# One product over 384 columns for a head's turn in place of three over 128, in a fused attention and mixture-of-experts kernel

## The chip, the cores and the metric

The kernel runs on one core of a Trainium2 chip. The metric is the device time of one launch in microseconds, from several runs; lower is better. One more execution was recorded by the profiler, and all rows below come from it.

## The reference

Attention with a threshold, then experts whose outputs are all summed with weights:

```
scores = scale * (q @ k.T)                      # 4 batches, 8 heads, 576 x 64
thresh = max(scores, -1) - tau
scores = where(scores >= thresh, scores, -1e9)
attn = exp(scores - max(scores))
attn = attn / (sum(attn) + 1e-9)
x = (attn @ v) -> 2304 tokens x 512             # heads side by side
p = probs / (sum(probs) + 1e-9)                 # 2304 x 4
out = sum over e of p[:, e] * (relu(x @ w1[e]) @ w2[e])   # 512 -> 1024 -> 512
```

All inputs and the output are float32.

## The kernel before

**Tokens in chunks.** The 2304 tokens are cut into chunks of 384, 640, 640 and 640. For each chunk the attention is computed for all 8 heads, and then four experts run over it. Attention of the first chunk runs alone; that of a later chunk runs among the experts' products of the chunk before it.

**Units.** Heads are taken in pairs; each head of a pair is a turn. The query rows of a pair are cut into units of 128, numbered through the whole kernel (131 of them). The first chunk has 4 pairs, 8 turns and 24 units, three for each turn (the code calls these pairs solid; `SOLID` is 24). The first 27 units (`LONE`) are done before the first expert product is allowed to start.

**Steps of a unit.** `s`: scores on TensorE (L767, L768) into one of two PSUM places (before unit 27: `s_ps` and `e_ps` by turns). `max` on DVE (L973), `thr` on ACT (L886), `exp` on ACT (L892) into one of three SBUF tiles `p`, `mask` on DVE (L979) with the sum, `eps` on POOL (L724), `rec` on DVE (L984), `norm` on POOL (L732, L734). `tr`: five transposes on TensorE into the single tile `t_ps` (L779). `phi`: a copy of it on ACT. From the second chunk on it is rounded to fp32r (L903), and `plo` on DVE (L989, L994) makes the rest that the rounding left, so that products run as several fp32r products of high and low parts (`pv`, L806, L808). In the first chunk `phi` copies whole fp32 numbers (L899), and the product with v is one of whole fp32 numbers (`pv32`, L791). When all of a pair's units are done, `x_hi` on ACT (L916) rounds the sum and `x_lo32` on DVE (L1006) makes the rest.

**The first chunk's values.** After each unit, `pv32` makes five products of 128 columns, one for each 128 keys, into that unit's columns of `x_ps`. The v tiles of two turns (`v32`) and two copies of turned tiles (`pt32`) lie in the space of `acc`, the output accumulator, which isn't in use yet. A copy waits until the values of the unit two before it are done.

**Experts.** A group "up" (L833 to L835) makes 128 rows of h for up to 384 or 320 columns with 12 matmuls; "down" (L847 to L849) makes 128 tokens of output in two halves of 12 matmuls. The weights come in 256 pieces of 128x512 (16 for each expert and chunk), through three stage buffers into a ring of 12: `w_hi` on ACT (L936), the low part on POOL (`wlo`, L745) or for every fourth piece on DVE (L1011). A down group needs all eight pieces of its half of the expert's weights.

**The order.** Each engine's queue is a list written at build time. `timeline()` gives every step a due time: for the steps of a unit the unit's time plus an offset from `ALONE` (the first 27 units) or `AMONG` (all later ones); `PLAN` has the time between units while attention is alone (`period`), when the experts start after it, and when the first 12 weight pieces are due. `settle()` then goes through time with a duration for each step (`TAKES`) and what it depends on (`follows()`), and gives each free engine the step with the earliest due time among those whose inputs are there. The chip runs this order with semaphores.

Of the kernel before, what the change touches and what calls it, by code (L numbers as in the profile page):

```python
# [5 lines left out]
F32 = mybir.dt.float32  # L6
# [5 lines left out]
P = 128  # L12
# [7 lines left out]
PAD = QT * P  # L20
# [80 lines left out]
def last_unit(turn):  # L101

    pair = PAIRS[turn // 2]
    return pair.first + pair.units - 1 if turn % 2 else pair.last_a
# [83 lines left out]
def ups_through(t, f):  # L188
# [4 lines left out]

ALONE = dict(load=-8.77, q_hi=7.33, q_lo=8.92, k_hi=-2.19, k_lo=-9.69, v_hi=1.58, v_lo=-4.93, max=5.2, thr=10.67,
             exp=8.87, mask=7.67, eps=5.66, rec=3.23, norm=13.37, tr=0.02, phi=3.52, plo=4.35, pv=8.26, xo=11.33,
             xs=0.95, x_hi=4.53, x_lo=9.85)
AMONG = dict(load=-9.42, q_hi=-0.79, q_lo=2.54, k_hi=-4.78, k_lo=-8.73, v_hi=-0.48, v_lo=-0.66, max=-2.12, thr=-0.54,
             exp=1.35, mask=1.63, eps=-4.19, rec=4.86, norm=3.57, tr=6.16, phi=8.2, plo=10.73, pv=10.67, xo=7.94,  # L200
             xs=13.36, x_hi=11.44, x_lo=12.33)
PLAN = dict(first=3.68, period=3.6, experts=11.97, end=12.63, weights=23.82, weight=7.74, prob=20.69)


def halves_of(u):
# [16 lines left out]
def timeline():  # L222

    steps = []

    def add(t, name, *x):
        steps.append((t, len(steps), name, x))

    def mm(count, n):
        return count * max(n * 0.00043 + 0.009, 0.111)  # L230

    def unit(t, u, at):
        pair = UNIT_PAIR[u]
        add(t, "s", u)
        for name in ("max", "thr", "exp", "mask", "eps", "rec", "norm"):
            add(t + at[name], name, u)
        for half in halves_of(u):
            for name in ("tr", "phi") if pair.solid else ("tr", "phi", "plo"):
                add(t + at[name] + 0.1 * half, name, u, half)
        if pair.solid:  # L240
            add(t + at["pv"], "pv32", u)
        for side, first in enumerate((pair.first, pair.first_b)):
            if u == first:
                turn = 2 * pair.index + side
                add(t + at["load"], "k_load", turn)
                add(t + at["load"] + 0.1, "q_load", turn)
                add(t + at["load"] + 4, "v32_load" if pair.solid else "v_load", turn)
                for name in ("k_hi", "k_lo", "q_hi", "q_lo") + (() if pair.solid else ("v_hi", "v_lo")):
                    add(t + at[name], name, turn)
        for part in pair.parts:  # L250
            if part.unit == u:
                for name in ("pv", "xo", "xs"):
                    add(t + at[name], name, part)
        if u == pair.first + pair.units - 1:
            add(t + at["x_hi"], "x_hi", pair)
            add(t + at["x_lo"], "x_lo32" if pair.solid else "x_lo", pair)

    for u in range(LONE):
        unit(PLAN["first"] + PLAN["period"] * u, u, ALONE)
    t = PLAN["first"] + PLAN["period"] * (LONE - EARLY) + PLAN["experts"]  # L260
    add(PLAN["prob"], "prob", 0)
    up_end, down_end = {}, {}
    units = list(range(LONE, UNITS))
    for c, (n, _, _) in enumerate(CHUNKS):
        todo = []
        for g in (g for g in GROUPS if g.c == c):
            if g.kind == "up":
                todo.append((mm(12, g.cols[1]), "up", g))
            else:
                todo += [(mm(12, D), "down", g, half) for half in range(2)]  # L270
        here = sum(UNIT_PAIR[u].c == c + 1 for u in units)
        space = (sum(s[0] for s in todo) - PLAN["end"]) / max(here, 1)
        done, next_unit = 0.0, 0.0
        for cost, name, *x in todo:
            if here and done >= next_unit:
                next_unit += space
                here -= 1
                unit(t, units.pop(0), AMONG)
                t += 1.7
            add(t, name, *x)  # L280
            t += cost
            done += cost
            g = x[0]
            if name == "up":
                add(t + 0.1, "hhi", g)
                add(t + 0.75, "hlo", g)
                up_end[g.t, g.j] = t
            elif x[1] == 1:
                add(t + 0.1, "acc", g)
                down_end[g.t] = t  # L290
                if g.e == E - 1:
                    add(t + 0.9, "store", g)
        assert not here
    when = PLAN["weights"]
    for m in range(len(CHUNKS) * E * PIECES):
        if m < RING:
            when += PLAN["weight"]
        else:
            to, i = divmod(m - RING, PIECES)
            free = up_end[to, i] if i < FT else down_end[to]  # L300
            when = max(when + 1.3, free + 0.1)
        add(when - 3, "w_load", m)
        add(when, "whi", m)
        add(when + 0.7, "wlo_dve" if lo_on_dve(m) else "wlo", m)
    return steps
# [7 lines left out]
              q_lo="DVE", max="DVE", mask="DVE", rec="DVE", plo="DVE", xs="DVE", x_lo32="DVE", hlo="DVE", acc="DVE", wlo_dve="DVE", prob="DVE")  # L313
TAKES = dict(q_load=1.2, k_load=1.2, v_load=1.2, v32_load=1.2, w_load=0.6, store=0.6,
             k_lo=1.45, v_lo=0.9, thr=0.22, eps=0.22, norm=1.1, wlo=1.32,
             pv32=1.1, down=2.75, k_hi=0.68, v_hi=0.47, exp=0.75, whi=0.63,
             max=0.76, mask=0.9, rec=0.17, acc=0.76, wlo_dve=0.93, prob=3.6)

TURNS_TAKE = dict(tr=(0.8, 0.25, 0.53), phi=(0.6, 0.28, 0.71), plo=(0.69, 0.29, 0.98))
# [27 lines left out]
def follows(name, x, half=2):  # L347
# [6 lines left out]
    if name in ("q_load", "k_load", "v_load"):  # L354
        return [(name[0] + "_lo", x - 1)] if x else []
    if name == "v32_load":
        return [("pv32", last_unit(x - 2))] if x >= 2 else []
    if name == "pv32":
        pair = UNIT_PAIR[x]
        return ([("phi", x, 2), ("v32_load", 2 * pair.index + (x >= pair.first_b))]  # L360
                + ([("x_lo32", PAIRS[pair.index - 2])] if pair.index >= 2 else []))
    if name == "x_lo32":
        return [("x_hi", x)]
    if name in ("q_hi", "k_hi"):
# [15 lines left out]
            return [("norm", x), ("phi", x - 1, 2)]  # L380
        return [("norm", x)] + ([("plo", x - 1, half) if x < LONE else whole("plo", x - 1)] if x else [])
    if name == "phi" and x < SOLID:
        return [("tr", x, 2)] + ([("pv32", x - 2)] if x >= 2 else [])
    if name == "phi":
        return [("tr", x, half)] + ([("pv", PARTS[parts_before(x) - 1])] if parts_before(x) else [])
    if name == "plo":
# [8 lines left out]
    if name == "xs":  # L395
        return [("xo", x)]
    if name == "x_hi" and x.solid:
        return [("pv32", x.first + x.units - 1)]
    if name == "x_hi":
        return [("xs", x.parts[-1])] + ([("up", UP_GROUPS[UPS_TO[(x.c - 1) * E - 1] - 1])] if x.c >= 2 else [])  # L400
    if name == "x_lo":
# [104 lines left out]
def build(nc, qT, kT, v, tau, dp, w1, w2, out):  # L506
    ctx = ExitStack()
    with ctx:
        def sb(name, shape, dt=F32):
            return ctx.enter_context(nc.sbuf_tensor(name, shape, dt))  # L510
# [17 lines left out]
        w_hi = sb("w_hi", [P, RING, 512], F32R)  # L528
        w_lo = sb("w_lo", [P, RING, 512], F32R)
        stage = sb("stage", [P, STAGES, 512])  # L530
        h_hi = sb("h_hi", [P, FT, 640], F32R)
        h_lo = sb("h_lo", [P, FT, 640], F32R)
        acc = sb("acc", [P, 5, D])
# [38 lines left out]
        def pt_cols(u):  # L572
            return slice(pt_col(u), pt_col(u) + P)

        spare = acc[:].rearrange("p j d -> p (j d)")

        def v32(side):
            return spare[:, side * PAD:(side + 1) * PAD].rearrange("p (k n) -> p k n", n=P)  # L580

        def pt32(u):
            return spare[:, (2 + u % 2) * PAD:(3 + u % 2) * PAD].rearrange("p (k n) -> p k n", n=P)

        t_tile = t_ps[:, 0:PAD].rearrange("p (k n) -> p k n", n=P)
        TURNED = (slice(0, QT - 1), slice(QT - 1, QT), slice(0, QT))
# [54 lines left out]
        def _(sp):  # L641
# [3 lines left out]
            for name, x in ORDER:  # L645
# [16 lines left out]
                elif name == "v32_load":  # L662
                    turn, = x
                    src, to = v[head(turn)], v32(turn % 2)[:, :, main_rows(turn)]
                    if turn >= 2:
                        sp.wait_ge(s_pv32, last_unit(turn - 2) + 1)
                    else:
                        sp.wait_ge(s_zero, 1)
                    sp.dma_start(to[:, 0:QT - 1, :], src[0:(QT - 1) * P, :].rearrange("(j p) d -> p j d", p=P)
# [30 lines left out]
        def _(pool):  # L700
            gp = nc.gpsimd
            gp.memset(ident[:], 1.0).then_inc(s_ident, 1)
            gp.memset(spare[:, 0:2 * PAD], 0.0).then_inc(s_zero, 1)
            gp.memset(q_hl[0][:, SEQ:PAD].bitcast(F32), 0.0).then_inc(s_zero, 1)
            gp.memset(q_hl[1][:, 0:PAD - SEQ].bitcast(F32), 0.0).then_inc(s_zero, 1)
            for i in range(P_BUFS):
# [42 lines left out]
        def _(pe):  # L749
# [3 lines left out]
            for name, x in ORDER:  # L753
# [25 lines left out]
                        op = nc.tensor.transpose(t_ps[:, tile], p[u % P_BUFS][:, tile], ident[:])  # L779
                    op.then_inc(s_tr, 1)  # L780
                elif name == "pv32":
                    u, = x
                    pair = UNIT_PAIR[u]
                    side, c0 = divmod((u - pair.first) * P, pair.n)
                    pe.wait_ge(s_phi, turned(u))
                    pe.wait_ge(s_v32_ld[side], (pair.index + 1) * 32)
                    if pair.index >= 2:
                        pe.wait_ge(s_xl, pair.index - 1)

                    for k in range(QT):  # L790
                        op = mm(x_ps[:, pair.index % 2, c0:c0 + P], v32(side)[:, k, :], pt32(u)[:, k, :],  # L791
                                start=u == pair.first and k == 0,
                                stop=u == pair.first + pair.units - 1 and k == QT - 1)
                    op.then_inc(s_pv32, 1)
                elif name == "pv":
                    part, = x
# [57 lines left out]
        def _(act):  # L854
# [6 lines left out]
            for name, x in ORDER:  # L861
# [31 lines left out]
                elif name == "phi":  # L893
                    u, half = x
                    act.wait_ge(s_tr, turned(u, half))
                    if u < SOLID:
                        if u >= 2:
                            act.wait_ge(s_pv32, u - 1)
                        run(pt32(u), t_tile, copy).then_inc(s_phi, 1)  # L899
                        continue  # L900
                    if parts_before(u):
# [9 lines left out]
                elif name == "x_hi":  # L911
                    pair, = x
                    c0 = pair.x_col
                    if pair.solid:
                        act.wait_ge(s_pv32, pair.first + pair.units)
                        run(x_hi[:, pair.k, c0:c0 + pair.n], x_ps[:, pair.index % 2, 0:pair.n], copy).then_inc(s_xh, 1)  # L916
                        continue
                    act.wait_ge(s_xs, pair.parts[-1].index + 1)
# [139 lines left out]
```

## Time and profile before

| what | value |
|---|---|
| median of 3 runs | 1117.29 us (1116.6 to 1117.81) |
| time of the profiled execution | 1117.18 us |
| its span, first to last instruction | 1115.4 us |
| mean granted TensorE clock | 0.998 |
| TensorE matmul busy | 1083.8 us (97%) |
| weight loads busy | 999.1 us (90%) |
| DVE, ACT, POOL busy | 611.4, 575.5, 636.9 us |

Busy times are sums of the recorded durations of an engine without overlaps. Matmuls are pipelined: each is recorded longer than its distance to the next, so the distance between two starts says what one costs. The first chunk's attention fills about the first 83 us, the experts' products all the rest.

### The profile page before, as it was taken

How to read it: one execution, taken by the hardware profiler on the slowest of the kernel's cores; microseconds unless marked ns; L12 is line 12 of the kernel's file. 1: busy time of each engine (PE TensorE's matmuls, PEld its weight loads, DVE VectorE, ACT ScalarE, POOL GpSimd, SP SyncE). 2: the span in 40 equal slices, each digit the busy share in tenths (PEclk: the TensorE clock that was granted, in tenths of full speed). 3: DMA queues.
4: the chain of work that ended last, by engine and by line, in shares of the span. 5: the costliest groups of instructions: out<-in, count | busy, mean ns of one | idle time of the engine just before them, and what ended most of it. 6: DMA issues, size and time to landing. Idle time of an engine off the chain costs nothing.

```text
span 1115.4 us, 18769 instructions
## 1 busy us (share of the span) xinstructions
PE 1083.8 (97%) x6628; PEld 999.1 (90%) x6628; DVE 611.4 (55%) x1268; ACT 575.5 (52%) x1173; POOL 636.9 (57%) x788
## 2 busy tenths in 40 slices
PE   5899999999899999999999999999999999999998
PEld 4889899998798898999989989989899898989897
DVE  5878777777665664765654557656466221212121
ACT  6877666666673562744735636546356141414140
POOL 6868767677884672754747827638366152525240
PEclk9999999999999999999999999999999999999999
DMA  5534443434453331431324513314223141313121
GB/s 153 156 92 110 125 128 102 144 90 144 127 154 101 83 112 36 111 99 50 99 92 136 167 53 104 103 26 122 66 64 89 39 114 48 105 47 107 46 85 48
DMA packets 95644, 108.10 MB, mean 97 GB/s; under 512 B 47168, under 2 KB 51264, under 8 KB 95552
## 3 DMA queue, kind: packets, MB, share of 16 engines
q1 hardware_dynamic: 95248, 106.57, 33.5%
q8 instruction: 54, 0.88, 0.3%
q10 hardware_dynamic: 304, 0.33, 0.1%
q14 instruction: 38, 0.31, 0.1%
HBM read 102.14 MB, written 4.72 MB: 96 GB/s over the span
## 4 chain that ended last, share of the span: by engine, by line
PE 84%; DVE 4%; POOL 4%; DMA 3%; ACT 2%; issue 2%; SPq 1%; ACTq 0%; DVEq 0%
PE e_ps L849 11%; PE e_ps L847 11%; PE e_ps L848 11%; PE e_ps L833 10%; PE e_ps L835 10%; PE e_ps L834 10%; PE t_ps L779 6%; PE s_ps L767 3%; PE x_ps L806 3%; PE s_ps L768 3%; PE x_ps L808 2%; POOL w_lo L745 2%; DMA stage<-w 1%; DVE neg_m L973 1%; PE x_ps L791 1%
## 5 line engine op out<-in xcount | busy, mean ns | idle before, releaser
L745 POOL TENSOR_TENSOR w_lo<-stage,w_hi 128x512 fp32r<-128x512 f32 x240 | 314.7, 1315 | 193.8 <-ACT w_hi L936 190.6
L833 PE MATMUL e_ps<-x_hi,w_hi 128*128 128x320 f32 (+1 forms) x896 | 286.0, 319 | 2.3 <-DVE h_lo L1017 2.3
L835 PE MATMUL e_ps<-x_hi,w_lo 128*128 128x320 f32 (+1 forms) x896 | 280.9, 313 | 0.0
L834 PE MATMUL e_ps<-x_lo,w_hi 128*128 128x320 f32 (+1 forms) x896 | 280.7, 313 | 0.0
L936 ACT ACTIVATE w_hi<-stage 128x512 fp32r<-128x512 f32 x256 | 158.1, 625 | 140.6 <-PE e_ps L849 96.8
L847 PE MATMUL e_ps<-w_hi,h_hi 128*128 128x512 f32 x576 | 228.0, 396 | 0.0
L849 PE MATMUL e_ps<-w_hi,h_lo 128*128 128x512 f32 x576 | 225.3, 391 | 0.0
L848 PE MATMUL e_ps<-w_lo,h_hi 128*128 128x512 f32 x576 | 224.7, 390 | 0.0
L1017 DVE SCALAR_TENSOR_TENSOR h_lo<-e_ps,h_hi 128x320 fp32r<-128x320 f32 (+1 forms) x224 | 111.7, 499 | 122.1 <-ACT h_hi L926 120.2
L833 PEld LDWEIGHTS e_ps<-x_hi,w_hi 128*128 128x128 f32 x896 | 168.9, 189 | 3.7 <-DVE h_lo L1017 3.5
L834 PEld LDWEIGHTS e_ps<-x_lo,w_hi 128*128 128x128 f32 x896 | 169.0, 189 | 0.2
L835 PEld LDWEIGHTS e_ps<-x_hi,w_lo 128*128 128x128 f32 x896 | 168.8, 188 | 0.0
L926 ACT ACTIVATE h_hi<-e_ps 128x320 fp32r<-128x320 f32 (+1 forms) x224 | 98.8, 442 | 103.3 <-PE e_ps L835 101.6
L979 DVE SCALAR_TENSOR_TENSOR p<-s_ps,thr,p 128x576 f32<-128x576 f32 x131 | 107.0, 817 | 51.4 <-ACT p L892 45.6
L849 PEld LDWEIGHTS e_ps<-w_hi,h_lo 128*128 128x128 f32 x576 | 108.1, 188 | 23.6
L848 PEld LDWEIGHTS e_ps<-w_lo,h_hi 128*128 128x128 f32 x576 | 108.3, 188 | 19.9
L903 ACT ACTIVATE pt_hi<-t_ps 128x640 fp32r<-128x640 f32 (+1 forms) x123 | 84.7, 689 | 80.2 <-PE t_ps L779 77.6
L847 PEld LDWEIGHTS e_ps<-w_hi,h_hi 128*128 128x128 f32 x576 | 108.2, 188 | 19.7
L973 DVE TENSOR_REDUCE neg_m<-s_ps 128x1 f32<-128x576 f32 x131 | 98.8, 754 | 48.1 <-PE s_ps L768 46.7
L734 POOL TENSOR_SCALAR p<-p,inv 128x576 f32<-128x576 f32 x144 | 109.1, 758 | 14.0 <-DVE inv L984 2.5
L715 POOL TENSOR_TENSOR k_ll<-k_raw,k_hh 128x576 fp32r<-128x576 f32 x56 | 81.6, 1458 | 54.3 <-ACT k_hh L876 53.4
L724 POOL TENSOR_SCALAR total<-total 128x1 f32<-128x1 f32 x144 | 31.8, 221 | 136.5 <-DVE p L979 130.1
(63 smaller groups left out, 1562.2 us busy)
## 6 DMA issues: line engine op xcount, KB each, us to landing
stage<-w SPq DMA_DIRECT2D x256, 256.0 KB, 2.8
k_raw<-kT SPq DMA_DIRECT2D x110, 144.0 KB, 2.9
v_raw<-v SPq DMA_DIRECT2D x48, 128.0 KB, 2.2
out<-acc SPq DMA_DIRECT2D x18, 256.0 KB, 2.0
q_raw<-qT SPq DMA_DIRECT2D x16, 144.0 KB, 2.8
q_raw<-qT SPq DMA_DIRECT2D x16, 128.0 KB, 2.7
q_raw<-qT SPq DMA_DIRECT2D x16, 112.0 KB, 2.7
q_raw<-qT SPq DMA_DIRECT2D x16, 96.0 KB, 2.7
```

The lines of the kernel that those rows point to most:

```text
L734: gp.tensor_scalar(tile, tile, col(inv, u), 1.0, ALU.mult, ALU.mult).then_inc(s_norm, 1)
L745: gp.tensor_tensor(w_lo[:, m % RING, :], stage[:, m % STAGES, :], w_hi[:, m % RING, :], ALU.subtract).then_inc(s_wl, 1)
L833: mm(ps[:, 0:n], w_hi[:, piece, tile], x_hi[:, k, cols], start=k == 0, stop=False)
L834: mm(ps[:, 0:n], w_hi[:, piece, tile], x_lo[:, k, cols], start=False, stop=False)
L835: op = mm(ps[:, 0:n], w_lo[:, piece, tile], x_hi[:, k, cols], start=False, stop=k == KT - 1)
L847: mm(ps, h_hi[:, f, tile], w_hi[:, piece, :], start=f == 0, stop=False)
L848: mm(ps, h_hi[:, f, tile], w_lo[:, piece, :], start=False, stop=False)
L849: op = mm(ps, h_lo[:, f, tile], w_hi[:, piece, :], start=False, stop=f == FT - 1)
L936: run(w_hi[:, m % RING, :], stage[:, m % STAGES, :], copy).then_inc(s_wh, 1)
L973: ve.tensor_reduce(col(neg_m, u), s_slot(u), AX.XY, ALU.max, negate=True).then_inc(s_max, 1)
L979: ve.scalar_tensor_tensor(out=tile, in0=s_slot(u), scalar=col(thr, u), in1=tile, op0=ALU.is_ge, op1=ALU.mult, accum_out=col(total, u)).the ...
L1017: ve.scalar_tensor_tensor(out=h_lo[:, g.j, c0:c0 + n], in0=e_ps[:, g.bank, 0:n], scalar=0.0, in1=h_hi[:, g.j, c0:c0 + n], op0=ALU.max, op1 ...
```

## The change

The first chunk's products with v are made once for each turn instead of once for each unit: five products over 384 columns, three units side by side, each unit's columns read from its own tile. Six copies of turned tiles are kept instead of two, three for each of two turns. They and the two v tiles lie in a tensor named `solid`, which is given the space of `h_hi` (the experts' hidden values, first written after the first up group) and no longer that of `acc`. A copy of unit u (from unit 6 on) waits for the product of the turn before the last one; the load of v and `x_hi` wait for turns instead of units. In the planner `pv32` is one step with the turn's last unit and takes 3.4 in place of 1.1, and all due-time offsets and constants of the plan are new, so that the order of steps on every engine, for the whole kernel, can be another.

```diff
-ALONE = dict(load=-8.77, q_hi=7.33, q_lo=8.92, k_hi=-2.19, k_lo=-9.69, v_hi=1.58, v_lo=-4.93, max=5.2, thr=10.67,
-             exp=8.87, mask=7.67, eps=5.66, rec=3.23, norm=13.37, tr=0.02, phi=3.52, plo=4.35, pv=8.26, xo=11.33,
-             xs=0.95, x_hi=4.53, x_lo=9.85)
-AMONG = dict(load=-9.42, q_hi=-0.79, q_lo=2.54, k_hi=-4.78, k_lo=-8.73, v_hi=-0.48, v_lo=-0.66, max=-2.12, thr=-0.54,
-             exp=1.35, mask=1.63, eps=-4.19, rec=4.86, norm=3.57, tr=6.16, phi=8.2, plo=10.73, pv=10.67, xo=7.94,
-             xs=13.36, x_hi=11.44, x_lo=12.33)
-PLAN = dict(first=3.68, period=3.6, experts=11.97, end=12.63, weights=23.82, weight=7.74, prob=20.69)
+ALONE = dict(load=-17.5, q_hi=5.39, q_lo=7.64, k_hi=-0.46, k_lo=-9.81, v_hi=1.71, v_lo=-2.54, max=9.79, thr=12.41,
+             exp=9.37, mask=8.96, eps=6.14, rec=3.8, norm=13.97, tr=-0.89, phi=1.36, plo=2.2, pv=5.08, xo=13.86,
+             xs=-0.75, x_hi=5.12, x_lo=7.64)
+AMONG = dict(load=-9.47, q_hi=-2.06, q_lo=1.61, k_hi=-4.55, k_lo=-7.63, v_hi=0.51, v_lo=1.44, max=-2.64, thr=0.17,
+             exp=1.23, mask=0.93, eps=-2.18, rec=4.43, norm=1.8, tr=6.54, phi=8.04, plo=8.73, pv=10.77, xo=7.6,
+             xs=10.2, x_hi=13.81, x_lo=10.72)
+PLAN = dict(first=3.17, period=3.99, experts=12.48, end=12.47, weights=24.2, weight=10.36, prob=24.14)
...
-        if pair.solid:
-            add(t + at["pv"], "pv32", u)
+        if pair.solid and u in (pair.last_a, pair.first + pair.units - 1):
+            add(t + at["pv"], "pv32", 2 * pair.index + (u > pair.last_a))
...
-             pv32=1.1, down=2.75, k_hi=0.68, v_hi=0.47, exp=0.75, whi=0.63,
+             pv32=3.4, down=2.75, k_hi=0.68, v_hi=0.47, exp=0.75, whi=0.63,
...
     if name == "v32_load":
-        return [("pv32", last_unit(x - 2))] if x >= 2 else []
+        return [("pv32", x - 2)] if x >= 2 else []
...
     if name == "phi" and x < SOLID:
-        return [("tr", x, 2)] + ([("pv32", x - 2)] if x >= 2 else [])
+        return [("tr", x, 2)] + ([("pv32", x // 3 - 2)] if x >= 6 else [])
...
+        with nc.sbuf_tensor("solid", [P, FT, PAD], F32) as solid:
+            pass
         h_hi = sb("h_hi", [P, FT, 640], F32R)
...
-        spare = acc[:].rearrange("p j d -> p (j d)")
-
         def v32(side):
-            return spare[:, side * PAD:(side + 1) * PAD].rearrange("p (k n) -> p k n", n=P)
+            return solid[:, side, :].rearrange("p (k n) -> p k n", n=P)

         def pt32(u):
-            return spare[:, (2 + u % 2) * PAD:(3 + u % 2) * PAD].rearrange("p (k n) -> p k n", n=P)
+            return solid[:, 2 + u % 6, :].rearrange("p (k n) -> p k n", n=P)
+
+        def pt32_turn(turn, k):
+
+            first = 2 + turn % 2 * 3
+            return solid[:, first:first + 3, k * P:(k + 1) * P]
...
                 elif name == "pv32":
-                    u, = x
-                    pair = UNIT_PAIR[u]
-                    side, c0 = divmod((u - pair.first) * P, pair.n)
-                    pe.wait_ge(s_phi, turned(u))
+                    turn, = x
+                    pair, side = PAIRS[turn // 2], turn % 2
+                    pe.wait_ge(s_phi, turned(last_unit(turn)))
                     pe.wait_ge(s_v32_ld[side], (pair.index + 1) * 32)
                     if pair.index >= 2:
                         pe.wait_ge(s_xl, pair.index - 1)
-
+                    ps = x_ps[:, pair.index % 2, 0:pair.n].rearrange("p (u n) -> p u n", n=P)
                     for k in range(QT):
-                        op = mm(x_ps[:, pair.index % 2, c0:c0 + P], v32(side)[:, k, :], pt32(u)[:, k, :],
-                                start=u == pair.first and k == 0,
-                                stop=u == pair.first + pair.units - 1 and k == QT - 1)
+                        op = mm(ps, v32(side)[:, k, :], pt32_turn(turn, k), start=side == 0 and k == 0,
+                                stop=side == 1 and k == QT - 1)
                     op.then_inc(s_pv32, 1)
...
                     if u < SOLID:
-                        if u >= 2:
-                            act.wait_ge(s_pv32, u - 1)
+                        if u >= 6:
+                            act.wait_ge(s_pv32, u // 3 - 1)
                         run(pt32(u), t_tile, copy).then_inc(s_phi, 1)
```

## Rows read from the trace of the kernel before

**Rows 1.** The page: busy time, and TensorE's busy tenths in 40 slices.

```profile
PE 1083.8 (97%) x6628; PEld 999.1 (90%) x6628; DVE 611.4 (55%) x1268; ACT 575.5 (52%) x1173; POOL 636.9 (57%) x788
...
PE   5899999999899999999999999999999999999998
```

**Rows 2.** Busy time by stretch, with granted clock, DMA share, GB/s.

```profile
0.00:8.20 8.20, 0.01 (x1) 0.04 (x1) 1.81 (x6) 3.54 (x6) 3.92 (x14) 1.00 0.59 135
8.20:16.80 8.60, 4.67 (x16) 4.00 (x17) 6.01 (x12) 5.02 (x11) 5.93 (x8) 1.00 0.62 162
16.80:83.30 66.50, 60.57 (x466) 56.04 (x465) 51.61 (x119) 53.44 (x105) 48.17 (x67) 1.00 0.47 130
83.30:1115.40 1032.10, 1018.55 (x6149) 939.06 (x6147) 551.95 (x1133) 513.45 (x1052) 578.91 (x701) 1.00 0.33 94
...
300.00:304.00 4.00, 4.00 (x29) 4.00 (x29) 1.90 (x7) 2.44 (x7) 3.72 (x7) 0.93 0.28 65
```

**Rows 3.** TensorE's timeline at 66 us, and from 77 us: start, duration.

```profile
66.33 0.71 PE L779 MATMUL t_ps<-ident,p 128*128 128x128 f32 x5
66.88 2.40 PE L791 MATMUL x_ps<-acc 128*128 128x128 f32 x20
69.11 0.71 PE L779 MATMUL t_ps<-ident,p 128*128 128x128 f32 x5
...
77.03 0.30 PE L767 MATMUL e_ps<-k_hh,q_hl 128*128 128x288 f32 x1
...
77.57 0.71 PE L779 MATMUL t_ps<-ident,p 128*128 128x128 f32 x5
```

**Rows 4.** TensorE's waits: the product's in the first 90 us, then all after.

```profile
PE x_ps L791 <- ACT acc L899: 2.4, 4, 0.8
...
PE t_ps L779 <- POOL p L734: 3.4, 3, 2.2
PE e_ps L833 <- DVE h_lo L1017: 2.3, 3, 1.1
PE s_ps L767 <- DVE p L979: 2.1, 4, 0.8
PE x_ps L806 <- DVE pt_hi L994: 2.0, 2, 1.8
PE s_ps L767 <- POOL k_ll L715: 0.2, 1, 0.2
```

**Rows 5.** Groups by line in 16.8 to 83.3 us: TensorE, then ACT.

```profile
L791 PE MATMUL x_ps<-acc 128*128 128x128 f32 x240 | 30.6, 279 | 2.4 <-ACT acc L899 2.4
L779 PE MATMUL t_ps<-ident,p 128*128 128x128 f32 x125 | 19.2, 287 | 1.8 <-POOL p L734 1.1 <-ACT acc L899 0.4
...
L899 ACT ACTIVATE acc<-t_ps 128x640 f32<-128x640 f32 x24 | 16.8, 701 | 6.5 <-PE t_ps L779 6.2
```

**Rows 6.** TensorE's timeline: two neighbouring rounded products over 384 columns.

```profile
83.52 0.34 PE L834 MATMUL e_ps<-x_lo,w_hi 128*128 128x384 f32 x1
83.69 0.34 PE L835 MATMUL e_ps<-x_hi,w_lo 128*128 128x384 f32 x1
```

**Rows 7.** Groups by line in the first 130 us: steps of a unit, one memset.

```profile
L979 DVE SCALAR_TENSOR_TENSOR p<-s_ps,thr,p 128x576 f32<-128x576 f32 x22 | 17.9, 815 | 6.2 <-ACT thr L886 3.0 <-ACT p L892 3.0
L973 DVE TENSOR_REDUCE neg_m<-s_ps 128x1 f32<-128x576 f32 x23 | 17.3, 754 | 5.1 <-PE s_ps L768 4.7
...
L724 POOL TENSOR_SCALAR total<-total 128x1 f32<-128x1 f32 x35 | 8.7, 248 | 16.6 <-DVE p L979 14.7
...
L984 DVE RECIPROCAL inv<-total 128x1 f32<-128x1 f32 x35 | 5.5, 161 | 5.8 <-POOL total L724 5.1
...
L703 POOL MEMSET acc<- 128x1280 f32 x1 | 1.2, 1165 | 0.0
```

**Rows 8.** The timeline at the end of the alone stage, all engines.

```profile
79.82 2.40 PE L791 MATMUL x_ps<-acc 128*128 128x128 f32 x20
...
82.25 0.49 ACT L916 ACTIVATE x_hi<-x_ps 128x384 fp32r<-128x384 f32 x1 [0.53 <-PE x_ps L791]
...
82.78 0.56 DVE L1006 TENSOR_TENSOR x_lo<-x_ps,x_hi 128x384 fp32r<-128x384 f32 x1
...
83.34 0.34 PE L833 MATMUL e_ps<-x_hi,w_hi 128*128 128x384 f32 x1
```

**Rows 9.** POOL's and TensorE's timelines around the first twelve weight pieces' end.

```profile
54.76 1.28 POOL L745 TENSOR_TENSOR w_lo<-stage,w_hi 128x512 fp32r<-128x512 f32 x1
...
91.81 1.43 POOL L715 TENSOR_TENSOR k_ll<-k_raw,k_hh 128x576 fp32r<-128x576 f32 x1 [0.45 <-ACT k_hh L876]
...
112.36 0.39 PE L847 MATMUL e_ps<-w_hi,h_hi 128*128 128x512 f32 x1
```

More of the change, by code:

```diff
@@ L356, in follows @@
     if name == "v32_load":
-        return [("pv32", last_unit(x - 2))] if x >= 2 else []
+        return [("pv32", x - 2)] if x >= 2 else []
     if name == "pv32":
-        pair = UNIT_PAIR[x]
-        return ([("phi", x, 2), ("v32_load", 2 * pair.index + (x >= pair.first_b))]
-                + ([("x_lo32", PAIRS[pair.index - 2])] if pair.index >= 2 else []))
+        return ([("phi", last_unit(x), 2), ("v32_load", x)]
+                + ([("x_lo32", PAIRS[x // 2 - 2])] if x >= 4 else []))
     if name == "x_lo32":
@@ L397, in follows @@
     if name == "x_hi" and x.solid:
-        return [("pv32", x.first + x.units - 1)]
+        return [("pv32", 2 * x.index + 1)]
     if name == "x_hi":
@@ L665, in _ @@
                     if turn >= 2:
-                        sp.wait_ge(s_pv32, last_unit(turn - 2) + 1)
+                        sp.wait_ge(s_pv32, turn - 1)
                     else:
@@ L702, in _ @@
             gp.memset(ident[:], 1.0).then_inc(s_ident, 1)
-            gp.memset(spare[:, 0:2 * PAD], 0.0).then_inc(s_zero, 1)
+            gp.memset(solid[:, 0:2, :], 0.0).then_inc(s_zero, 1)
             gp.memset(q_hl[0][:, SEQ:PAD].bitcast(F32), 0.0).then_inc(s_zero, 1)
@@ L914, in _ @@
                     if pair.solid:
-                        act.wait_ge(s_pv32, pair.first + pair.units)
+                        act.wait_ge(s_pv32, 2 * pair.index + 2)
                         run(x_hi[:, pair.k, c0:c0 + pair.n], x_ps[:, pair.index % 2, 0:pair.n], copy).then_inc(s_xh, 1)
```

## The prediction, made before the changed kernel was run

> **What bounds the kernel now.** I read the page first, then the busy time by stage, then TensorE's waits, then single stretches. The page gives TensorE as busy for 97% of the span, and the slices show that it is so from the third slice on [rows 1]. That figure hides gaps, since the end of a matmul is modelled. The Trainium skill (Perfetto Trace Analysis, Identifying the Most-Contended Engine) likewise calls matmul busy time a bad measure; the trace agrees, and so I count from start to start.
>
> The stages [rows 2]: up to 16.8 us the engines fill; from 16.8 to 83.3 us the first chunk's attention runs alone; then the experts' products run, with the later chunks' attention among them. In the alone stage no engine is full: of 66.5 us DVE works 51.6, ACT 53.4, POOL 48.2. From start to start, scores of one unit take 77.57 − 77.03 = 0.54 us, transposes 66.88 − 66.33 = 0.55 us, and values of two units 69.11 − 66.88 = 2.23 us, so 1.115 each [rows 3]. The stage holds 25 units' scores, 125 transposes and 24 units' values [rows 5], so 25 × 1.09 + 24 × 1.115 = 54.0 us: TensorE has 12.5 us of room in 66.5. A unit takes 66.5 / 24 = 2.77 us, and the length is set by handing a unit from engine to engine, with ACT (53.4 / 24 = 2.23 us a unit) nearest to its limit. After that stage TensorE sets the end: apart from what it works it waits 10.0 us in all (3.4 + 2.3 + 2.1 + 2.0 + 0.2) [rows 4]. So two things can be won: hand-over time before 83.3 us, and those 10.0 us.
>
> **The products.** Removed: 24 steps of 5 products over 128 columns (240 records, two for each product [rows 5]), 24 × 1.115 = 26.8 us. Added: 8 steps of 5 products over 384 columns, 80 records. The trace has no whole fp32 product of that width. From below: a rounded fp32 matmul of 384 columns follows its neighbour after 83.69 − 83.52 = 0.17 us [rows 6], which gives 80 × 0.17 = 13.9 us (0.174 unrounded over the twelve of one group) and saves 12.9. From above: columns cost what they cost now, 3 × 0.1115 = 0.335 us a record, 26.8 us, and nothing is saved. Which end? At 128 columns the spacing cannot tell: the transposes, one record for 128 columns, come every 0.55 / 5 = 0.11 us as well, so this may be a floor under any record and not the price of its columns. If a record streams its columns twice, 128 of them need 0.107 us at 2.4 GHz, which fits the 0.1115, and 384 need 0.320; with the 0.01 us that the rounded ones show above their own 0.16 that is 0.33 us, 26.4 us in all, 0.4 saved. The nearest row is that of the same instruction with the same types, so I take this value, and keep −12.9 and 0 as bounds. The Trainium skill (FP8 and Floating Point Precision, TensorE Precision Notes) has true fp32 make four passes through the array. By it a product is 4 × 384 columns, 0.64 us, hence 25.6 us in all at least, and the wider form saves at most 1.2 us; no run here shows that width yet. Term: **−0.4 us**.
>
> **The waits of these products.** Values of a unit wait for the copy of its turned tile (phi). TensorE stood 2.4 us in four such waits [rows 4]. With a third as many steps and six copies kept, two of three units need no such moment. But one still comes after the last copy of a turn, and an idle moment of an engine with 12.5 us of room is only partly time. Term: **−1.0 us** (bounds 0 and −2.4). The other relief, that a copy no longer waits for the values two units before, is worth nothing: of the 6.5 us for which ACT stood idle before copies, 6.2 ended on the transposes and none on the values [rows 5].
>
> **The burst.** One step now holds TensorE for 3.3 us where steps of 1.1 us stood, though the old order already put two together for 2.23 us in places [rows 3]. Behind it in TensorE's queue stand scores and transposes. Their users: DVE has 0.75 + 0.82 + 0.16 = 1.73 us a unit (maximum, mask, reciprocal [rows 7]), and two banks of scores hold 3.5 us of work for it, so 3.3 us are covered if both are full when the burst begins; three softmax tiles do the same for POOL and for the transposes after. Term 0, and +1.5 us for each of seven bursts that begins with only one bank full (3.3 − 1.7, rounded down for the part of a head's q that it has to do as well), before what the room takes back. At the end nothing covers it: the last pair of units' values ran 79.82 to 82.05, x_hi at 82.25, x_lo at 82.78, first expert product at 83.34 [rows 8]. Now three units follow the last copy, so the last x is 1.1 us later; the transposes and scores that filled the gap fill it already, and the first group can start on the earlier three parts of x. Term: **+1.1 us** (bounds 0 and +1.1).
>
> **Memory.** Tiles that lay in acc lie where h comes later. The first write to h follows the first up group, which waits for x anyway; acc's first use is later still. The clearing before was one memset of 1.2 us during the fill [rows 7], and is one of the same size. The values' DMAs keep their number and size, and wait for the same turn's end, so SP's queue gets no new wait. All nothing; the copies keep their size and their 0.70 us [rows 5].
>
> **The order.** The due times of every step are new, and all queues are ordered by them, so this touches the 1032 us after the alone stage too. In the among part, normalising is due 1.8 us after the scores where it was 3.57, the low part of the turned tile at 8.73 where it was 10.73. The two waits that these end are TensorE's for the normalised tile, 3.4 us, and for the turned tile, 2.0 us, 5.4 of the 10.0 [rows 4]. I take half, **−2.7 us**. Bounds: −10 us, all waits gone, and +6, as many again as these that I name, since moving attention earlier delays something else on the same queues. The half-speed stretch of the clock (granted 0.93 in 300 to 304 us [rows 2], so 0.3 us there) I leave: what sets it off can't be read from one row.
>
> **Sum.** −0.4 − 1.0 + 1.1 − 2.7 = −3.0 us. The profiled execution took 1117.18 us for a span of 1115.4, 0.1 us under the median of 1117.29, so the median becomes **1114.2 us**, 0.3% less. What a measurement here can tell from no change is about 0.2%, 2.2 us.
>
> **Rivals.**
> *It only shifts waits (chance 0.32).* The alone stage keeps 2.77 us a unit and the 10 us stay. For it: only 0.4 us of work is removed, and the whole gain that I expect is hand-over time, of which a rearranged order commonly takes as much elsewhere. Time: 1117.3 − 0.4 + 1.1 = 1118.0, within 1115.1 and 1119.5.
> *Weights late at the first down group (slower, 0.14).* The low part of piece 15, in the plan's clock, was due at 23.82 + 12 × 7.74 + 4 × 1.3 = 121.9, 19.9 us after the experts' start (3.68 + 24 × 3.6 + 11.97 = 102.0), and is now due at 24.2 + 12 × 10.36 + 5.2 = 153.7, 42.3 after theirs (111.4), while the first down group is planned 27 us after it (16.7 of up groups and six units at 1.7). Attention steps of three units (15 / 4.96 us) go ahead of it on POOL, at 0.25 us for the sum [rows 7] and at most the 1.43 us of a head's k part [rows 9] for each of normalising and the share of k and v, 3.1 us as an upper end; I take 2.6, so 8 us. Against it: the last of POOL's share of the first twelve pieces was done at 56.0 us, far ahead of its due time, and the first down group came only at 112.36 [rows 9]: pieces are made whenever an engine is free. If half of the 8 us is not filled by attention that runs ahead, with none of my gain in the order: 1118.0 + 4 = 1122. It decides once those low parts end after the eighth up group.
> *Bursts starve DVE (slower, 0.11).* If four of seven begin with one bank full: +6 us, a third taken back by the room: 1118.0 + 4 = 1122, and the alone stage ends after 87 us.
> *Columns at one pass a record (0.06).* The 12.9 us fall out of the alone stage's TensorE work, where it has room already; I count two thirds, 1117.3 − 8.6 = 1108.7.
> My forecast has 0.37. Faster: 0.37 + 0.06 = 0.43; same 0.32; slower 0.25. Its own range is 1111 to 1115: the order's term from −6 to −2. The range for 8 in 10: from 1108.5, just under the last rival's time, to 1121, which leaves out the worse half of the slower ones.
>
> **What would show it.** Records of the new products 0.33 us apart (0.17 would mean the last rival); a turn's step 3.3 us; first expert product between 82 and 84 us; TensorE's waits for normalised and turned tiles after 90 us under 3 us together; no wait of TensorE for w_lo. I am wrong if waits for DVE's masks grow in the alone stage, if w_lo appears as releaser of L847 to L849, or if the order moves the 10 us up instead of down: that is the term I know least.

## The result, and the profile after

The changed kernel took 1128.24 us (median of 4 runs, 1124.99 to 1131.28) against 1117.55 of the kernel before: 1.0% slower (ratio 1.0096, 95% interval 1.0067 to 1.0126). The profiled execution was the slowest of the four, 1131.28 us with a span of 1129.5, so its rows show some 3 us more loss than the median does.

Busy time by stretch of the changed kernel, PE, PEld, DVE, ACT, POOL, then granted clock, DMA share and GB/s; the second row is the alone stage, which ended at 83.3 us before [rows 2]:

```profile
0.00:17.07 17.07, 4.68 (x17) 4.03 (x18) 7.87 (x18) 8.49 (x16) 9.86 (x21) 1.00 0.59 146
17.07:98.81 81.74, 65.69 (x307) 47.32 (x305) 55.42 (x121) 54.98 (x107) 50.36 (x72) 0.94 0.38 108
98.81:1129.50 1030.69, 1017.38 (x6149) 939.03 (x6147) 551.13 (x1130) 513.64 (x1051) 574.25 (x697) 1.00 0.32 94
```

The whole loss lies before the first expert product: 98.81 against 83.34 us, +15.5. What follows took 1030.7 us against 1032.1. DVE, ACT and POOL did the same work as before within 4 us, in 15 us more. TensorE's waits in the alone stage (total, times, longest):

```profile
PE t_ps L783 <- ACT solid L901: 8.9, 6, 2.9
PE e_ps L771 <- DVE p L981: 4.1, 4, 2.3
PE x_ps L794 <- ACT solid L901: 1.8, 2, 1.0
PE t_ps L783 <- POOL p L738: 0.7, 2, 0.4
PE s_ps L771 <- DVE p L981: 0.6, 2, 0.3
```

16.1 us in place of 5.5. The product's own wait fell from 2.4 [rows 4] to 1.8. What grew is that *transposes* wait for the copy of the unit before them (8.9 us, 0.4 before) and scores for a mask (4.7 us, 1.6 before). One turn at full clock, all engines (start, duration):

```profile
72.26 0.82 DVE L981 SCALAR_TENSOR_TENSOR p<-e_ps,thr,p 128x576 f32<-128x576 f32 x1
...
72.96 3.39 PE L794 MATMUL x_ps<-solid 128*128 128x384 f32 x10
...
73.48 0.74 DVE L975 TENSOR_REDUCE neg_m<-s_ps 128x1 f32<-128x576 f32 x1
...
76.18 0.71 PE L783 MATMUL t_ps<-ident,p 128*128 128x128 f32 x5
...
76.65 0.38 PE L771 MATMUL e_ps<-k_hh,q_hl 128*128 128x288 f32 x1
...
77.49 0.75 DVE L975 TENSOR_REDUCE neg_m<-e_ps 128x1 f32<-128x576 f32 x1
...
77.78 0.74 PE L783 MATMUL t_ps<-ident,p 128*128 128x128 f32 x5
...
78.27 0.74 ACT L894 ACTIVATE p<-e_ps,neg_m 128x576 f32<-128x576 f32 x1 [0.63 <-DVE neg_m L975]
78.91 0.69 ACT L901 ACTIVATE solid<-t_ps 128x640 f32<-128x640 f32 x1
79.50 0.29 ACT L888 ACTIVATE thr<-neg_m,tau_col 128x1 f32<-128x1 f32 x1
...
79.75 0.74 PE L783 MATMUL t_ps<-ident,p 128*128 128x128 f32 x5 [1.23 <-ACT solid L901]
79.89 0.82 DVE L981 SCALAR_TENSOR_TENSOR p<-e_ps,thr,p 128x576 f32<-128x576 f32 x1 [0.99 <-ACT thr L888]
...
80.77 0.40 PE L771 MATMUL e_ps<-k_hh,q_hl 128*128 128x288 f32 x1 [0.28 <-DVE p L981]
...
81.41 0.81 PE L794 MATMUL x_ps<-solid 128*128 128x384 f32 x2
```

Read it from the second row. The product holds TensorE for 76.18 − 72.96 = 3.22 us. When it begins, one bank of scores is full, not two, since the mask of the first row still reads the other: DVE takes that maximum at 73.48 and has no other scores until those of 76.65. Then a chain starts: maximum 77.49, exponential 78.27, copy of a turned tile 78.91, threshold 79.50, mask 79.89, next scores 80.77, next product 81.41. A turn takes 81.41 − 72.96 = 8.45 us; the one wide product and 5.2 us of chain. DVE does not stand idle during the product, as the busy times of that stretch show:

```profile
72.96:76.18 3.22, 3.22 (x12) 1.85 (x11) 2.88 (x7) 1.96 (x4) 2.91 (x4) 1.00 0.00 0
```

DVE works 2.88 of the 3.22 us (in the other four products at full clock after the first turn's, 2.73 to 2.88), on one maximum, one mask and the low part of q. So the time is lost behind the product, not during it: the steps that need a second unit's scores start only after it, one behind the other. The transposes of 77.78 are done at once, but their copy stands on ACT behind the exponential of 78.27, so the next transposes wait 1.23 us. Before, from turn 2 to turn 7 the last unit's product moved from 43.84 to 80.94 us, 7.4 us a turn; here from 45.70 to 92.50, 9.4.

The rest is clock. TensorE at half speed, by stretch:

```profile
62.25:67.76 5.51, 5.51 (x15) 3.44 (x16) 4.10 (x9) 2.45 (x5) 3.92 (x7) 0.69 0.03 8
...
90.41:97.81 7.40, 7.40 (x20) 4.83 (x21) 3.87 (x10) 3.74 (x8) 4.37 (x9) 0.59 0.23 61
```

The first follows transposes that waited 1.43 us, the second transposes that waited 2.94. In the two, a wide product takes 4.49 and 5.31 us instead of 3.22. The first turn's product, at 23.50, took 5.38 us as well, though the clock column reads 1.00 there.

### The profile page after: what moved, and what is told of

Its sections match the earlier page's. It is cut to its first block, busy times and chain, and to the rows that moved or that the text cites. A ratio compares the mean times of both kernels' runs of the same rounds, so it can differ in the third digit from the quotient of the medians.

```text
span 1129.5 us, 18429 instructions
## 1 busy us (share of the span) xinstructions
PE 1087.8 (96%) x6468; PEld 990.4 (88%) x6468; DVE 614.4 (54%) x1268; ACT 577.1 (51%) x1173; POOL 634.5 (56%) x788
## 4 chain that ended last, share of the span: by engine, by line
PE 87%; DVE 4%; DMA 2%; issue 2%; ACT 2%; POOL 1%; SPq 1%; ACTq 0%; DVEq 0%
PE e_ps L849 11%; PE e_ps L851 11%; PE e_ps L850 11%; PE e_ps L835 11%; PE e_ps L836 10%; PE e_ps L837 10%; PE t_ps L783 6%; PE s_ps L771 3%; PE s_ps L772 3%; PE x_ps L808 3%; PE x_ps L794 3%; PE x_ps L810 3%; DMA stage<-w 2%; DVE p L981 1%; DVE q_hl L960 1%
## 5 line engine op out<-in xcount | busy, mean ns | idle before, releaser
L928 ACT ACTIVATE h_hi<-e_ps 128x320 fp32r<-128x320 f32 (+1 forms) x224 | 98.8, 442 | 109.0 <-PE e_ps L837 107.7
L975 DVE TENSOR_REDUCE neg_m<-s_ps 128x1 f32<-128x576 f32 x131 | 98.8, 754 | 52.7 <-PE s_ps L772 51.5
L783 PE MATMUL t_ps<-ident,p 128*128 128x128 f32 x720 | 105.4, 277 | 12.7 <-ACT solid L901 8.9
```

## The experiments

**Which part of the change?** Four kernels. First, the changed kernel with `ALONE`, `AMONG` and `PLAN` of the kernel before:

> The changed kernel with the due times of the kernel before (products over 384 columns stay one step a turn). Theory burst (one step that holds TensorE for 3.2 us puts the next scores, and everything queued behind them on ACT, late): the alone stage stays long, first expert product at 94 to 99 us, time 1122 to 1129. Theory plan (the new due times do the harm): back near the kernel before, first expert product at 83 to 86, time 1116 to 1120.

1133.39 us, ratio 1.0132 (1.0111 to 1.0153), first expert product at 99.36: the loss stays, and is larger than expected. Second, the kernel before with all the new constants:

> The kernel before with the new due times and nothing else of the change (products of 128 columns a unit, two copies in acc's space). Theory burst: first expert product at 82 to 86 us, time 1115 to 1120. Theory plan: first expert product after 92 us, time 1124 or more.

1121.49 us, ratio 1.0036 (1.0024 to 1.0048), first expert product at 85.08: the stage as theory burst had it, the time a little over. (Below, the number without a name behind a ratio is the first expert product.) Third, the same with six copies in h's space:

```diff
+            return solid[:, 2 + u % 6, :].rearrange("p (k n) -> p k n", n=P)
...
+                        if u >= 6:
+                            act.wait_ge(s_pv32, u - 5)
```

> The kernel before with the new due times, six copies of turned tiles kept, and these and v in h's space: all of the change but the wide product. Theory burst: as e2, 1115 to 1120. Theory memory or buffers (h's space or the looser wait does harm): over 1124, with e2 near 1117.

1122.13 us, ratio 1.0035 (1.0023 to 1.0047), 87.0. So the wide step costs with either set of constants: by the first expert product +16.0 us with the old ones (99.4 against 83.3) and +11.8 with the new ones (98.8 against 87.0), in time 16 and 6. The constants themselves cost some 4 us on a kernel with narrow products and save 5 on the wide one. Fourth, the turn's five products as steps of their own:

```diff
+            for k in range(QT):
+                add(t + at["pv"] + 0.01 * k, "pv32", 2 * pair.index + (u > pair.last_a), k)
...
+             pv32=0.68, ...
```

> The changed kernel with the five products of a turn as five steps of their own (0.65 us each), which the planner may put between scores and transposes. Same instructions in number and width. Theory burst: much of the loss comes back, first expert product at 84 to 89 us, no half-speed clock after the start, time 1115 to 1121. If the width itself (reading three tiles in one product) does the harm: products slower than 0.32 us a record, time stays over 1124.

1133.15 us, ratio 1.014 (1.0122 to 1.0158), 96.2: a miss. Cutting the step lets the planner write another order, and that order was no better; so this run does not say whether the length matters. The next ones therefore keep an order fixed.

**Fixed orders.** The kernel before's queues, with the turn's work where the last unit's step stood:

```diff
+def by_turn(order):
+    return [("pv32", (x[0] // 3,)) if name == "pv32" else (name, x) for name, x in order
+            if name != "pv32" or x[0] % 3 == 2]
+ORDER = by_turn(ORDER)
```

> Every engine's queue in the order of the kernel before, step for step; only TensorE's product of a turn is one wide step where the turn's last unit had its own, and the two earlier units' steps are gone. Memory as in the change. Theory lateness (a turn's work in one piece, 3.2 us long, behind which the next scores and transposes come late): first expert product at 90 us or later, time 1122 to 1130. Theory order (the planner's answer to a 3.4 us step, with two transposes in a row, does the harm, not the step): 84 to 87 us, time 1117 to 1120.

1133.26 us, ratio 1.0146 (1.013 to 1.0161), first expert product at 100.8: lateness, by more than expected. Here DVE does run dry: in the four products at full clock it works 1.03 to 2.72 of some 3.23 us. The same place, but narrow products:

> As the previous one, but the turn's work at that place is 15 products over 128 columns. Theory lateness: the same time as with wide ones within 1 us. If the wide form itself costs (three tiles read in one product), it is faster than the wide one by more than 2 us.

1132.77 us, ratio 1.0138 (1.0116 to 1.016), 97.8 (its profiled execution was 3 us under its median, the wide kernel's 1.5 above). Wide or narrow makes no difference that the times can tell; doing a turn's values in one piece does. The wide form itself is sound: ten records in 3.23 us, 0.323 each, the narrow thirty in 3.35. Now the changed order with narrow products, each right behind the next unit's transposes:

```diff
+        if name == "tr" and 0 < x[0] < SOLID and done < x[0]:
+            found.append(("pv32", (done,)))
+            done += 1
```

> Every queue in the order of the changed kernel, step for step; only the products are narrow ones of a unit, each put right behind the next unit's transposes (which wait for the same copy), at the latest where the wide step stood. So TensorE works on values while ACT copies. Theory lateness: most of the 15 us come back, first expert product at 84 to 89 us, time 1115 to 1121. Theory order: over 1124.

1127.76 us, ratio 1.0096 (1.0079 to 1.0113), 94.6: only 4 us of the stage came back, none of it in the median time. Even the 4 us may be chance: the profiled execution was the fastest of its four, that of the changed kernel the slowest, 4.9 us apart. The changed order is slow with narrow products too. To see by how much, four of five products were left out, in three orders:

```diff
-                    for k in range(QT):
+                    for k in range(1):
```

> The changed kernel with only the first of a turn's five wide products; the other four are left out (the output is not the reference's), the order of every queue stays. 2.58 us less in each of 8 turns, 20.7 in all. Theory burst on the chain (a turn's period in the alone stage is the burst, 3.2 us, plus a chain scores, maximum, exponential, copy, transposes, mask of some 5.2 us behind it): the turn's period falls from 8.45 to about 5.9 to 6.5 us, first expert product at 80 to 84 instead of 98.8. If another engine's work sets the period: over 7.6 us, and first expert product over 92.

> The kernel before with only the first of each unit's five narrow products, the other four left out (the output is not the reference's): 0.89 us less for each of 24 units, 21.4 in all, nearly the same work taken out as in the one before. If products lie beside other work there, as my prediction had it: first expert product from 83.3 to 76 to 80. If TensorE is on the chain there as well: below 70.

> The old order of every queue with the turn's step at its last unit's place, as in the run with that order and wide products, but with only the first of its five products; the other four are left out (the output is not the reference's). Theory length (under the old order the loss is a step of 3.2 us in one piece, nothing else): first expert product at 82 to 86 us where it was 100.8, time 1114 to 1119. Theory place (the turn's step costs because it waits for a later copy, however short): over 92 us.

| order of the queues | all five products | one of five | taken out of TensorE | clock, five and one |
|---|---|---|---|---|
| changed, a step a turn | 98.8 us, 1128.24 | 91.5 us, 1124.71 | 20.7 us | 0.94, 0.81 |
| before, a step a turn | 100.8 us, 1133.26 | 84.2 us, 1117.92 | 20.7 us | 0.92, 0.85 |
| before, a step a unit | 83.3 us, 1117.3 | 83.2 us, 1114.67 | 21.4 us | 1.00, 0.95 |

(First expert product, then time; the last column is the clock granted from 17 us to the first expert product.) The first two one-product kernels behaved differently. In the old order the step's length is nearly the whole loss: 16.5 of 17.4 us go with it. In the changed order only 7.3 go, which fits neither of its theories whole: the period of over 7.6 us came, 91.5 us is just under the 92. The third kernel is a miss: 76 to 80 us was expected, and taking 21.4 us of TensorE's work out moved nothing. So in the kernel before, other engines set the length of this stage. The comparison has one flaw: with the work gone, TensorE idles more and is granted less clock, which may hide a part of what the removal is worth, most of all in the changed order. The timeline of that kernel (changed order, one product) shows what is left:

```profile
68.78 0.81 PE L794 MATMUL x_ps<-solid 128*128 128x384 f32 x2
...
72.55 0.40 PE L771 MATMUL s_ps<-k_hh,q_hl 128*128 128x288 f32 x1 [1.17 <-DVE p L980]
...
75.60 0.74 PE L783 MATMUL t_ps<-ident,p 128*128 128x128 f32 x5 [1.71 <-ACT solid L900]
...
77.51 1.48 PE L794 MATMUL x_ps<-solid 128*128 128x384 f32 x2
```

A turn still takes 8.7 us, and the clock is hardly in it (0.97 granted from 68.78 to 77.51): what DVE and ACT did beside the long product now stands behind the short one, and second scores and second transposes wait for it. The last line of the table also bounds what could be won: with four fifths of these products gone, the kernel before is 2.6 us faster (ratio 0.9977, 0.9962 to 0.9993). Of that, its profile shows 0.2 us up to the first expert product. The rest lies behind it, where nothing was taken out and seven profiles of the old order took anything from 1029.6 to 1032.2 us.

**The clock.** Idle products (identity by identity, results unused) in the places where two transposes stand in a row:

```diff
+                    if behind == "tr" and 3 <= u < SOLID:
+                        pe.wait_ge(s_xl, UNIT_PAIR[u].index)
+                        for _ in range(10 if u == 23 else 4):
+                            mm(x_ps[:, (UNIT_PAIR[u].index + 1) % 2, 0:P], ident[:], ident[:], start=True, stop=True)
```

> The changed kernel with idle products (identity by identity, results unused) where two transposes stand in a row, 4 of them before the second (10 at unit 23), to be done while TensorE waits for the copy. Theory clock (the half-speed stretches after idle moments cost some 4 to 6 us): full clock from 28 us on, first expert product at 94 to 96, time 1122 to 1125. If the clock does not depend on these waits or the waits are all of the loss: 1127 to 1130.

1127.42 us, ratio 1.0096 (1.0081 to 1.0111), 97.1. The stretch at 62 us was gone, but the clock still fell early and at 91 us; the time can't be told from the changed kernel's. Then in all larger waits, from the first microseconds on:

> The changed kernel with idle products on TensorE in all its larger waits of the alone stage: 12 before the first scores, 4 and 5 before those of units 2 and 3, 7 and 5 before those of units 7 and 9, and 5 (12 at unit 23) before the second of two transposes in a row. Theory clock (half-speed stretches are worth 4 to 6 us of the loss): no half-speed stretch between 10 and 100 us, first expert product at 92 to 95 us, time 1121 to 1125. If waiting is nearly all of it: 96 to 99 us, 1126 to 1129, at full clock.

```profile
8.20:17.07 8.87, 5.53 (x40) 4.85 (x39) 5.95 (x14) 5.57 (x12) 6.21 (x8) 1.00 0.62 173
17.07:94.00 76.93, 70.14 (x402) 54.62 (x403) 58.15 (x125) 55.59 (x111) 50.75 (x72) 0.98 0.41 113
```

1123.36 us, ratio 1.0052 (1.0035 to 1.0069), first expert product at 91.6, granted clock 0.98 in the alone stage where it was 0.94 (0.84 from 17.07 to 24 us, 1.00 from 30 us on). So half speed is worth 7.2 of the 15.5 us in the profiles and 4.9 of the 10.7 in the medians; the other half is waiting. The medians are the better measure, since the changed kernel's profile was its slowest execution. (With all five products this stage is now as short as with one of five, 91.5 us at a clock of 0.81: so the 7.3 us above are not a clean price of the length in this order.) Of the 7.2 us, 2.8 are gained by the third turn's product (turn 2 in the count above, 42.89 us against 45.70), before the two stretches shown above. The same early idle products in the kernel before:

> The kernel before, with idle products (identity by identity, overwritten later) on TensorE while it waits for its first inputs: 12 before the first scores, 4 before unit 2's, 5 before unit 3's. If the clock rises from half speed earlier than at 20.7 us, the first units' scores, transposes and values take half as long: 1 to 3 us less, 1114.5 to 1116.5. If the chain of the first units runs over the other engines: 1117 to 1118.

1117.22 us, ratio 0.9995 (0.998 to 1.0009), 83.9. The first product with v came 2.1 us earlier (17.99 against 20.05) and nothing of it was left at the end: the first units' chain there runs over the other engines.

**The constants among the experts, and the memory.**

> The kernel before with the new due times of the steps among the experts alone (AMONG); the alone stage's and the plan's constants stay. My prediction's term for the order was -2.7 us: 1114 to 1116. If the new due times among the experts cost, as the narrow kernel with all new constants suggests (1121.5, of which only 1.7 us by the first expert product): 1119 to 1122.

1120.99 us, ratio 1.0034 (1.0019 to 1.0049), 83.7. TensorE's waits after that (total, times, longest):

```profile
PE s_ps L767 <- DVE p L979: 3.2, 5, 1.0
PE t_ps L779 <- DVE pt_hi L994: 2.7, 1, 2.7
PE e_ps L833 <- DVE h_lo L1017: 2.2, 4, 1.0
PE x_ps L806 <- DVE pt_hi L994: 2.0, 2, 1.8
PE t_ps L779 <- POOL p L734: 0.9, 1, 0.9
```

11.0 us against 10.0 [rows 4], in a part that took 1035.4 us against 1032.1. The wait for the normalised tile did fall, from 3.4 to 0.9, but transposes wait 2.7 us for a low part instead, at 165 us, and a half-speed stretch that the kernel before did not have follows it (granted clock 0.69 from 165 to 168 us). The waits alone make 1 us; how the rest divides was not separated.

> The kernel before with six copies of turned tiles instead of two, all in h's space, the looser wait of the copy, and the old due times; products stay narrow. The order of the queues is the old one, so both theories expect no difference: first expert product at 83 to 84 us, 1116.5 to 1118. If the memory's place costs: over 1119.

1116.84 us, ratio 0.9999 (0.9988 to 1.0009), 84.3: memory and buffers cost nothing and give nothing that can be told. None of the fifteen kernels beat the one before with the whole computation done.

## Why the prediction was wrong

Forecast 1114.2 us, measured 1128.24, outside 1108.5 to 1121.

**The products, −0.4: right in kind.** A record of 384 columns takes 0.323 us where I had 0.33, so the term was −1.0 us of TensorE's work at full clock (80 × 0.323 = 25.8 for 26.8). The Trainium skill (FP8 and Floating Point Precision, TensorE Precision Notes) has true fp32 make four passes through the array. With the prediction's 0.16 us for 384 columns at 2.4 GHz, four passes are 0.64 us a product, an estimate; the trace agrees, 0.646. But the third line of the table of one-product kernels shows that this work was not what set the stage's length, so even the 12.9 us of the last rival would hardly have come out of it.

**The waits of these products, −1.0: of the right size, −0.6, and beside the point.** I took a lone wait out and did not look at what the copy would now be queued behind. The transposes' waits for the copy, 0.4 us in the kernel before, became 8.9. They were in no term: I had the transposes covered by "three softmax tiles", but they all go into the single tile `t_ps`, and the next ones wait until ACT has copied it.

**The burst, term 0: the step that failed.** I wrote that 3.3 us are covered "if both are full when the burst begins", and priced the other case at 1.5 us a burst as a rival with a chance of 0.11. In the turn shown one bank is full. The second could not be: its mask ran until 73.08, after the product's start, and that mask needed an exponential and a threshold from ACT. With the time taken back that I assumed, the rival gave an alone stage that ends "after 87 us"; without half speed it ends at 91.6, with it at 98.8. Its condition came true, and my sign of being wrong with it: waits for DVE's masks grew from 1.6 to 4.7 us. Its mechanism did so only in part. DVE starves in the old order with the long step. In the changed kernel it worked through the product, and the larger wait was for ACT's copies. What I left out is that a fixed order lets nothing be taken back, that the chain scores, maximum, exponential, copy, threshold, mask runs behind the product and not beside it (3.22 + 5.23 = 8.45 us in the turn shown), and that longer waits cost clock. Put where the term 0 stood, the runs show 15.5 us in one profile and some 11 in the medians, about half of it waiting and half of it clock. The one-product kernels show the length as the loss in the old order (16.5 us); in the order written for the long step most of the loss is in the order, at the clocks that they were granted. The end term, +1.1, can't be separated from this.

**Memory, 0: right** (ratio 0.9999).

**The order, −2.7: wrong in sign where it can be measured alone, +3.8 us** (0.34% of 1117). I counted two waits that earlier due times would end; in that run one fell as I said, and another took its place. In the changed kernel itself neither ended: after 98.8 us TensorE waits 3.1 us for the normalised tile and 1.9 for the turned one, 5.0 of 10.1, where it was 5.4 of 10.0, and I had said under 3. The part after the alone stage took 1030.7 us against 1032.1, which is no difference: with the old order of that part seven profiles gave 1029.6 to 1032.2 us, with the changed kernel's five gave 1029.4 to 1033.1. So there the term was nothing that can be told. The two need not agree: the planner turned the same due times into another order of the queues for the narrow step than for the wide one.

**The rival of late weights: did not happen.** No trace has a wait of TensorE for w_lo. **That waits only shift (1118.0): wrong**, they grew.

**The room.** My general mistake was in the first part: 12.5 us in which TensorE does nothing is room for work in small pieces that can be put where it idles. It is not room for one step of 3.2 us ahead of what every other engine waits for. That small pieces fit is shown for the old order only; in the changed order they brought little back.

Left open: why the five separate pieces, which shorten every step, gave 96 us; their order was the planner's own, and no run kept another order fixed with them. How the loss divides in the changed kernel's other executions, which were up to 6 us shorter than the profiled one, was not seen either.

## What to carry to other kernels

Joining three small steps of an engine into one can cost its length to everyone queued behind it, even where that engine has nearly a fifth of its time free: count the work that the others hold when it begins, by banks and buffers, and follow their queues once round. Test a reordered schedule with the order held fixed and the disputed work left out; if the time stays, the order and not the work is the bound. Look at the granted clock of both, since leaving work out can lower it (here from 0.94 to 0.81). And before making a step cheaper, leave it out: here that won 2.6 us.

## What the runs showed of the hardware

- A rise in waiting was paid twice: in the profiles 8.3 us of longer alone stage at nearly full clock, and 7.2 us more while TensorE ran at 1.2 GHz, at the start and after waits of 1.43 and 2.94 us. Idle products in the waits kept it at 2.4 from 30 us on and gave 4.9 us of the median time back, at no cost that shows. The reverse was seen too: with four fifths of the products with v left out, the granted clock of the stage fell from 1.00 to 0.95 and from 0.94 to 0.81.
- In the first microseconds the clock column reads 1.00, but score records of 288 columns start 0.24 us apart, and 0.13 later: the spacing shows the lower level, the column does not.
- DVE's low part of q, 64x192, takes 0.42 us, but 1.50 where it starts just behind POOL's subtraction for k. It then ends 0.21 us after POOL's operation does (75.78 and 75.57), as if it had waited for it. The kernel before has the same where the two meet (1.11 us at 85.17, ending 0.20 us after POOL's). In the changed kernel they meet in five turns of the alone stage; whether this lengthened a turn was not tested. The first two rows below are that pair, the third is one with no such neighbour, all of the changed kernel:

```profile
74.17 1.40 POOL L719 TENSOR_TENSOR k_ll<-k_raw,k_hh 128x576 fp32r<-128x576 f32 x1
74.28 1.50 DVE L960 SCALAR_TENSOR_TENSOR q_hl<-q_raw,tau_col,q_hl 64x192 fp32r<-64x192 f32 x1
...
95.86 0.42 DVE L960 SCALAR_TENSOR_TENSOR q_hl<-q_raw,tau_col,q_hl 64x192 fp32r<-64x192 f32 x1
```
